# Linear part of a PReLU layer over two PSUM banks, its left-over rows as narrow matmuls, and another way out for the last chunk

## The reference

```python
# B, N, C, A, F = 2, 12480, 128, 49, 2048
a2k = sm(agents, k);  agent_v = a2k @ v        # 49 x 128 for each batch
q2a = sm(q, agents)                            # 12480 x 49
x = q2a @ agent_v
h = x @ w_in
g = np.maximum(h, 0.0) + alpha * np.minimum(h, 0.0)
out = g @ w_out
```

## Time and profile before

| | us |
|---|---|
| median of 3 runs | 926.45 |
| the profiled execution's own time | 928.37 |
| its span, first to last instruction | 926.3 |
| mean granted clock of TensorE | 0.994 |

### The profile page before, as it was taken

One profiled execution on the slowest core, in us unless ns is written; L12 is line 12 of the kernel. 1 busy time (PEld: TensorE's weight loads), 2 busy tenths in 40 slices (PEclk: granted clock), 3 DMA queues, 4 the chain that ended last, 5 costly groups with the idle time before them and its releaser, 6 DMA issues.

```text
span 926.3 us, 16063 instructions
## 1 busy us (share of the span) xinstructions
PE 911.4 (98%) x5642; PEld 490.7 (53%) x5642; DVE 626.2 (68%) x923; ACT 514.7 (56%) x695; POOL 108.6 (12%) x138
## 2 busy tenths in 40 slices
PE   7989999999999999999999999999999999999998
PEld 7874555555546556554445444444444444444443
DVE  3637666766777767767767676767667676767664
ACT  2425555556555565555556565656565555555554
POOL 5400101001001001001011010101010101010101
PEclk9979999999999999999999999999999999999999
DMA  8941322322223322211111111212121111111110
GB/s 288 335 155 50 93 67 61 99 58 71 77 72 92 100 71 91 66 38 57 35 39 53 38 58 35 58 35 58 34 59 35 51 41 50 44 42 51 31 32 22
DMA packets 67813, 65.75 MB, mean 71 GB/s; under 512 B 38528, under 2 KB 63424, under 8 KB 67520
## 3 DMA queue, kind: packets, MB, share of 16 engines
q1 hardware_dynamic: 67488, 65.19, 23.3%
q10 hardware_dynamic: 288, 0.06, 0.0%
HBM read 40.49 MB, written 12.78 MB: 58 GB/s over the span
## 4 chain that ended last, share of the span: by engine, by line
PE 94%; DMA 2%; issue 2%; SPq 1%; DVE 0%; ACT 0%; POOLq 0%; ACTq 0%
PE ps L588 55%; PE ps L571 18%; PE ps L578 7%; PE ps L552 3%; PE ps L430 2%; PE ps L598 2%; PE ps L753 2%; DMA kv_s<-kT 2%; PE ps L747 1%; SPq L295 1%; PE ps L533 1%; PE ps L454 0%; PE ps L508 0%; PE ps L461 0%; DVE r_lo L1162 0%
## 5 line engine op out<-in xcount | busy, mean ns | idle before, releaser
L1162 DVE SCALAR_TENSOR_TENSOR r_lo<-ps,r_hi 128x960 f16<-128x960 f32 x416 | 466.4, 1152 | 247.6 <-ACT r_hi L919 245.2
L919 ACT ACTIVATE r_hi<-ps 128x960 f16<-128x960 f32 x416 | 386.1, 967 | 174.3 <-PE ps L578 174.3
L588 PE MATMUL ps<-r_hi,w_hi 128*128 128x480 f16 x832 | 252.1, 369 | 0.6 <-DVE r_lo L1162 0.6
L588 PE MATMUL ps<-r_hi,w_lo 128*128 128x480 f16 x832 | 248.0, 366 | 0.0
L588 PE MATMUL ps<-r_lo,w_hi 128*128 128x480 f16 x832 | 240.8, 366 | 0.0
L571 PE MATMUL ps<-PT,M_a 128*128 128x480 f16 x832 | 203.2, 366 | 0.5 <-DVE M_a L1114 0.3
L415 POOL TENSOR_TENSOR y<-y_relu,y_lin 128x480 f32<-128x480 f32 x52 | 62.3, 1199 | 614.8 <-ACT y_relu L1000 442.5
L588 PEld LDWEIGHTS ps<-r_hi,w_lo 128*128 128x128 f16 x832 | 91.2, 110 | 68.8
L571 PEld LDWEIGHTS ps<-PT,M_a 128*128 128x128 f16 x832 | 81.1, 99 | 86.7 <-DVE r_lo L1162 2.1
L588 PEld LDWEIGHTS ps<-r_lo,w_hi 128*128 128x128 f16 x832 | 85.4, 106 | 71.2
L588 PEld LDWEIGHTS ps<-r_hi,w_hi 128*128 128x128 f16 x832 | 73.2, 106 | 81.7 <-issue 39.2
(11 more groups left out here) (149 smaller groups left out, 521.1 us busy)
## 6 DMA issues: line engine op xcount, KB each, us to landing
q_s<-qT SPq DMA_DIRECT2D x52, 240.0 KB, 2.6
out<-y SPq DMA_DIRECT2D x52, 240.0 KB, 2.0
kv_s<-kT SPq DMA_DIRECT2D x24, 512.0 KB, 4.2
kv_s<-vP SPq DMA_DIRECT2D x12, 512.0 KB, 8.7
kv_s<-vS SPq DMA_DIRECT2D x8, 768.0 KB, 4.4
PR<-PT SPq DMA_DIRECT2D x156, 32.0 KB, 1.8
PT<-stack SPq DMA_TRANSPOSE x208, 2.3
w_lin<-w_out SPq DMA_DIRECT2D x1, 1024.0 KB, 8.2
```

What stands on the lines that cost most here:

```text
L588: mm = pe.matmul(ps[:, OUT, 0:CHUNK], w[:, 2 * p + u, :], r[:, s, u, :], start=(p == 0 and u == 0 and k == 0), stop=(p == PAIRS - 1 and u ...
L919: act.activation(r_hi[:, p % RING, :, :], ps[:, at:at + 2, 0:CHUNK], ACT.Relu).then_inc(hi_ready, 1)
L1162: dve.scalar_tensor_tensor(out=r_lo[:, p % RING, :, :], in0=ps[:, at:at + 2, 0:CHUNK], scalar=0.0, in1=r_hi[:, p % RING, :, :], op0=ALU.ma ...
```

## The change

The linear part goes to two banks. `linear` now has two matmuls by L_a, of two tiles (240 columns) each, into banks 0 and 1. L_b has 64 partitions, the 19 left-over rows at 0 and again at 32 (so mix_linear makes them twice, into two column groups), and no zero rows. A new `rest_of_linear`, behind the fourth group's rest_of_quad, adds L_b by two matmuls of 32 rows and 240 columns, one on row group 0 (from PT, bank 0) and one on row group 1 (from PR, bank 1). lin_ready comes from the second of these, SP's turn waits for it, and ScalarE's y_lin stands behind relu_hi of pair 6. For the last chunk ScalarE's y_relu and GpSimd's sum are left out: VectorE computes y from PSUM and y_lin in two halves, the first stored from SP's queue and the second from ScalarE's.

```diff
--- before.py
+++ after.py
@@ -14,6 +14,7 @@
 CHUNK = 4 * T
+HALF = CHUNK // 2
 WIDE = 128
@@ -109,8 +110,8 @@
         L_a = sb("L_a", [128, B, C], F16)
-        L_b = sb("L_b", [128, B, C], F16)
-        L_rh = sb("L_rh", [32, C], F16)
+        L_b = sb("L_b", [64, B, C], F16)
+        L_rh = sb("L_rh", [64, C], F16)
         out_unscale = sb("out_unscale", [128, B, 1])
@@ -181,8 +182,8 @@
         h_ready, hi_ready, lo_ready, pair_done = sem("h_ready"), sem("hi_ready"), sem("lo_ready"), sem("pair_done")
-        lin_ready, lin_saved, relu_saved, y_ready = (
-            sem(x) for x in ("lin_ready", "lin_saved", "relu_saved", "y_ready"))
+        lin_ready, lin_saved, relu_saved, y_ready, last_y = (
+            sem(x) for x in ("lin_ready", "lin_saved", "relu_saved", "y_ready", "last_y"))
@@ -280,14 +281,14 @@
-                groups = QUADS * n - QUADS
+                parts = n - 1
                 if not isinstance(n, int):
-                    groups = sp.compute_val(groups)
+                    parts = sp.compute_val(parts)
                 sp.wait_ge(stack_zero, 1)
                 if read is not None:
-                    sp.wait_ge(h_ready, groups)
+                    sp.wait_ge(lin_ready, parts)
                 sp.wait_ge(q_hi, n + 1)
@@ -336,20 +337,25 @@
                         spread(n + 2, half)
-
-                    sp.wait_ge(y_ready, n + 1)
-                    sp.dma_start(out[n], y[:, half, :]).then_inc(stored[half], 16)
+                    if there(n + 1):
+
+                        sp.wait_ge(y_ready, n + 1)
+                        sp.dma_start(out[n], y[:, half, :]).then_inc(stored[half], 16)
+                    else:
+
+                        sp.wait_ge(last_y, 1)
+                        sp.dma_start(out[n][:, 0:HALF], y[:, half, 0:HALF]).then_inc(stored[half], 16)
             each_body(sp, body)
-            for half in range(2):
-                sp.wait_ge(stored[half], 16 * BODIES)
+
+            sp.wait_ge(stored[0], 16 * BODIES + 16)
+            sp.wait_ge(stored[1], 16 * BODIES)
         @block.gpsimd
...
             pool.memset(gate[:, :], -1.0).then_inc(pool_step, 1)
             pool.memset(ones[:, :], 1.0).then_inc(consts, 1)
-            pool.memset(L_b[:, :, :], 0.0).then_inc(consts, 1)
             pool.memset(av_acc[:, :], 0.0).then_inc(consts, 1)
...
@@ -419,7 +425,8 @@
                         query_again(n + 2)
-                    finish(n, half, i)
+                    if there(n + 1):
+                        finish(n, half, i)
@@ -543,8 +550,9 @@
                 pe.wait_ge(b_avl, b + 1)
-                pe.matmul(ps[0:32, bank, C:2 * C], av_l[:, b, 128:SEL], lin_w[:, :], start=True, stop=True,
-                          skip_group_check=True)
+                for g in (0, 32):
+                    pe.matmul(ps[g:g + 32, bank, C:2 * C], av_l[:, b, 128:SEL], lin_w[:, :], start=True, stop=True,
+                              skip_group_check=True)
                 pe.matmul(ps[:, bank, 0:C], av_l[:, b, 0:128], lin_w[:, :], start=True, stop=True,
@@ -593,10 +601,18 @@
+
             def linear(half, b):
-                for w, end in ((L_a, False), (L_b, True)):
-                    mm = pe.matmul(by_tile(ps[:, 2 * LIN_SLOT, 0:CHUNK]), w[:, b, :], tokens(PT, half), start=not end,
-                                   stop=end)
+                for h in range(2):
+                    pe.matmul(by_tile(ps[:, 2 * LIN_SLOT + h, 0:HALF]), L_a[:, b, :], tokens(PT, half)[:, 2 * h:2 * h + 2, :],
+                              start=True, stop=False)
+
+
+            def rest_of_linear(half, b):
+                for h, src in enumerate((PT, PR)):
+                    at = slice(32 * h, 32 * h + 32)
+                    mm = pe.matmul(by_tile(ps[:, 2 * LIN_SLOT + h, 0:HALF]), L_b[at, b, :],
+                                   tokens(src[at, :, :], half)[:, 2 * h:2 * h + 2, :], start=False, stop=True)
                 mm.then_inc(lin_ready, 1)
...
@@ -819,6 +835,7 @@
                     rest_of_quad(3, half, b)
+                    rest_of_linear(half, b)
                     second_layer(4, half)
@@ -893,7 +910,7 @@
                 act.activation(L_a[:, b, :], ps[:, LIN_BANK[b], 0:C], ACT.Copy)
-                act.activation(L_rh[:, :], ps[0:32, LIN_BANK[b], C:2 * C], ACT.Copy).then_inc(l_high, 1)
+                act.activation(L_rh[:, :], ps[0:64, LIN_BANK[b], C:2 * C], ACT.Copy).then_inc(l_high, 1)
@@ -976,13 +993,14 @@
                     relu_hi(g + 5, quad + 2, 5, False)
+                    relu_hi(g + 6, quad + 3, 6, False)
                     act.wait_ge(lin_ready, n + 1)
                     if not (isinstance(i, int) and i == 0):
                         act.wait_ge(y_ready, n - 1)
-                    act.activation(y_lin[:, half, :], ps[:, 2 * LIN_SLOT, 0:CHUNK], ACT.Copy,
+                    act.activation(y_lin[:, half, :].rearrange("p (h n) -> p h n", n=HALF),
+                                   ps[:, 2 * LIN_SLOT:2 * LIN_SLOT + 2, 0:HALF], ACT.Copy,
                                    scale=lin_unscale[:, b, :]).then_inc(lin_saved, 1)
-                    relu_hi(g + 6, quad + 3, 6, False)
                     relu_hi(g + 7, quad + 3, 7, False)
@@ -996,9 +1014,14 @@
-                    act.wait_ge(pair_done, g + PAIRS)
-                    act.activation(y_relu[:, half, :], ps[:, OUT, 0:CHUNK], ACT.Copy,
-                                   scale=out_unscale[:, b, :]).then_inc(relu_saved, 1)
+                    if there(n + 1):
+                        act.wait_ge(pair_done, g + PAIRS)
+                        act.activation(y_relu[:, half, :], ps[:, OUT, 0:CHUNK], ACT.Copy,
+                                       scale=out_unscale[:, b, :]).then_inc(relu_saved, 1)
+                    else:
+
+                        act.wait_ge(last_y, 2)
+                        act.dma_start(out[n][:, HALF:CHUNK], y[:, half, HALF:CHUNK]).then_inc(stored[1 - half], 16)
@@ -1122,7 +1145,7 @@
                                          in1=ps[96:128, LIN_BANK[b], 0:C], op0=ALU.mult, op1=ALU.add)
-                dve.tensor_tensor(L_b[0:32, b, :], ps[0:32, LIN_BANK[b], C:2 * C], L_rh[:, :], ALU.subtract).then_inc(l_low, 1)
+                dve.tensor_tensor(L_b[:, b, :], ps[0:64, LIN_BANK[b], C:2 * C], L_rh[:, :], ALU.subtract).then_inc(l_low, 1)
...
@@ -1309,6 +1332,15 @@
                         relu_lo(g + 9, 1)
+                    else:
+
+                        dve.wait_ge(lin_saved, n + 1)
+                        dve.wait_ge(pair_done, g + PAIRS)
+
+                        dve.wait_ge(stored[half], 16 * i)
+                        for at in (slice(0, HALF), slice(HALF, CHUNK)):
+                            dve.scalar_tensor_tensor(out=y[:, half, at], in0=ps[:, OUT, at], scalar=out_unscale[:, b, :],
+                                                     in1=y_lin[:, half, at], op0=ALU.mult, op1=ALU.add).then_inc(last_y, 1)
```

More of the change, by code:

```diff
@@ L381, in over_channels @@
                 return x[:, :].rearrange("p (t o) -> p t o", o=1).to_broadcast(by_feature)
-            pool.wait_ge(consts, 5)
+            pool.wait_ge(consts, 4)
             pool.tensor_tensor(turn_sign[:, :, :], ident[:, :].rearrange("p (o c) -> p o c", o=1).to_broadcast(by_feature),
@@ L607, in _ @@
                 if m == FULL - 1:
-                    pe.wait_ge(consts, 5)
+                    pe.wait_ge(consts, 4)
                     relu_max_row()
@@ L1175, in _ @@
             dve.memset(v_tail[:, 0, 0:RUN + 1:RUN], 1.0).then_inc(ones_in, 1)
-            dve.wait_ge(consts, 5)
+            dve.wait_ge(consts, 4)
             for g in (0, 64):
```

## The result

The changed kernel takes 920.27 us (median of 6 runs, 918.06 to 923.07) against 926.74 (6 runs, 925.45 to 927.1): a ratio of 0.9933, 95% interval 0.9916 to 0.9951, so 6.2 us faster (4.5 to 7.8). Of all runs reported here one took far longer, the kernel with y_lin last once with 1482.32 us at a mean granted clock of 0.558, and the ratios leave it out.

What follows compares the result with a forecast made beforehand. The prediction took TensorE, busy 98% of the span, to bound the kernel. It summed -4.3 + 3 x 0.11 + 0.2 + 0.2 - 1.2 = -4.8 us, to 921.7 us for the median, range 920.5 to 927.3.

Steps and rivals of the forecast that it cites:

- tail and streaming at their good ends: Low end of the forecast range, 920.5 us: the last chunk's finish and the streaming both at their favourable bounds.
- mix_linear: One more 32-wide fp32 matmul, twice in the program, on TensorE's full path: +0.2 us (0.2 to 0.7).
- The shortened pair: Linear matmuls of each chunk: two L_a matmuls of 240 columns replace two of 480, saving 0.20 us a chunk.
- B: Rival: in each chunk the second L_a load sticks out by 0.05 us, +2.4 in all, 924.1; chance 0.10.
- The appended pair: Two L_b matmuls behind the fourth group's rest: loads hidden, side by side, 0.11 us a chunk (0.10 to 0.42).
- A: Rival: the L_b pair's loads wait until the four M_r matmuls have streamed, 0.21 us a chunk, 926.9; chance 0.15.
- C: Rival: the two L_b matmuls run one after the other, 0.31 us a chunk, 932.0, slower; chance 0.09.
- The four chunks that wait: Chunks where M_a's load waits for VectorE's r_lo: the 0.20 us saved is lost, +0.11 in three of them.
- y_lin: ScalarE's y_lin, moved behind r_hi of pair 6: nothing in ordinary chunks (0.7 us slack), +0.2 us in the last.
- D: Rival: the new order makes y_lin or pair 7's r_lo late in ordinary chunks; 0.1 us late gives 926.5; chance 0.04.
- The mix_rest row: Profile row of 16 narrow fp32 matmuls in 1.71 us, 0.107 each, taken to show same-shape narrow loads are hidden.
- The tail: After the last matmul: VectorE's two halves let the last store issue at 922.6 against 923.82, -1.2 us (-0.9 to -1.5).

## Why the prediction was right

The mechanism held step by step, and each rival's mark is absent. The size was short by 1.4 us, every term on the same side, which carried the median 0.2 us out of the range at its low end (920.5, "tail and streaming at their good ends"): mix_linear's bounds started at 0.2, and it cost nothing, and the pair was held to cost no less than 0.10, where a chunk gained 0.107 and not 0.10. *The shortened pair*: 0.20, as forecast; the second L_a load does not stick out (B). *The appended pair*: 0.10 against 0.11; its loads start over busy row groups (against A), the two run side by side (against C). With the plain chunk at 15.53, 48 ordinary chunks give 48 x -0.107 = -5.1 instead of -4.3: the largest part of what the forecast lacked, and a matter of 0.017 us a chunk. *The four chunks that wait*: +0.10 in three of them instead of +0.11; the loads of M_a wait 2.9 us for r_lo in 4 places where it was 2.1:

```profile
PEld ps L579 <- DVE r_lo L1185: 2.9, 4, 0.9
```

The 0.8 more is the 4 x 0.20 saved ahead of them. In ordinary chunks the prediction set r_lo against the start of the third M_a matmul and found 0.17 us left; against its load nothing is left. In the changed kernel's trace r_lo ends at 708.62 and that load starts at 708.68, 0.03 later than the stream would have it, and its matmul (708.85) doesn't move. *y_lin*: no new wait in ordinary chunks (against D), and in the last chunk one wait on r_lo; its cost there with the pair's was 0.10, not 0.20, because the matmul starts with its late load, not 0.11 behind it, and so stays 0.20 behind the one before. *mix_linear* was mis-sized, and its row misread: 0.2 was added, and it is near nothing. Where the second batch's pieces are made, L546 stood 0.33 us ahead of the next line:

```profile
496.32 0.41 PE L546 MATMUL ps<-lin_w,av_l 128*32 128x128 f32 x2
496.65 0.49 PE L548 MATMUL ps<-lin_w,av_l 128*128 128x128 f32 x2
```

And now, with one matmul more:

```profile
492.85 0.41 PE L554 MATMUL ps<-lin_w,av_l 128*32 128x128 f32 x4
493.19 0.49 PE L556 MATMUL ps<-lin_w,av_l 128*128 128x128 f32 x2
```

that is 0.34: two matmuls in different column groups stream side by side. The mix_rest row was read as one after the other. Its 32 instructions start four at a time, the fours 0.21 us apart, and at the 1.2 GHz level: a window on it in the kernel before shows a granted clock of 0.50.

```profile
67.40:69.10 1.70, 1.70 (x33) 1.56 (x33) 0.76 (x1) 0.60 (x1) 0.00 (x0) 0.50 0.00 0
```

So 0.107 us was neither the price of one nor a measure at the clock of the chunks. That narrow loads of one shape are hidden was forecast from it and is true, but it is shown by the chunk's own trace and by the kernel with one row group, not by that row. *The tail*: -1.4 instead of -1.2. The halves took 0.84, the store was issued 0.98 behind the last matmul instead of 0.83, and the smaller store landed in 1.8 us instead of 2.0 to 2.1, which pays for it.

Put together with measured terms: -5.1 + 3 x 0.10 + 0.1 + 0.0 - 1.4 = -6.1, the -6.08 of the traces and the -6.2 of the times.

The Trainium skill ("TensorE: Matmul & The Clock Gate", The mechanism) lets a load overlap matmuls in flight only where its row group differs. Here both L_b loads start at 709.36, 0.01 us into four matmuls on all row groups, and nothing of them sticks out: the measurement decides against that rule. The same section of the Trainium skill also lets a load into the background weight buffer be pulled ahead, and with that the trace agrees. The rule of the Trainium skill ("TensorEngine Tiling (Array Packing)", Key Properties) that a change of mode drains the array and a change of tile doesn't agrees with 0.32 us for the pair by itself and 0.10 in the narrow stretch. These rows don't tell a drain from a load that is waited for: at each change the load starts late, and the matmul with it.

## What to carry to other kernels

A narrow matmul on a few row groups costs its streaming alone where narrow ones already stand, and costs three times as much by itself: 0.10 against 0.32 us for the same pair, because each change of height costs about 0.11 us again. Spread it over row groups with a bank each; here the second row group was the whole gain. And before an instruction is moved on a helping engine, find its slot: one place earlier or later cost 0.09 and 0.18 us a plain chunk, where the change had won 0.11.

## What the runs showed of the hardware

A load of 98 ns hides behind 240 columns (0.10 us), in each of the 52 chunks (two L_a matmuls take 0.20 us where one of 480 columns took it); in a longer run of such halves about 3 ns stick out for each. A load may go into a row group while a narrow matmul streams through it (L_b's at 709.36, the quartet from 709.35). The start of this program varied by 4 us between traces (first linear matmul at 81.02 to 84.99), the earliest with the highest granted clock between 45 and 85 us (0.91) and the latest with the lowest (0.83); from there on the traces of one kernel agree within 0.01 us, and so settle what the times can't.
